# A drain in every expert tile, the row gather ahead of the scale lookup, and the last router block moved

## Chip, core and metric

The kernel runs on one core of a Trainium2 chip. The metric is device time in microseconds (us) for one execution; several executions are taken and their median is given. PE is TensorE, DVE is VectorE, ACT is ScalarE, POOL is GpSimd and SP is SyncE.

## What is computed

Three stages in a row over 2304 tokens of width 512. An attention with features is followed by a gated network, and that by a network of 8 experts of which each token uses one:

```python
def _moe_ref(x, w_gate, w_val, w_out):
    g = x @ w_gate
    silu = g * (1.0 / (1.0 + np.exp(-g)))
    return (silu * (x @ w_val) @ w_out).astype(np.float32)

def _moe2_ref(x, w_gate, w_output_gate, w1, w2):
    logits = x @ w_gate
    e_idx = np.argmax(logits, axis=1)
    ...   # gate_w: the chosen expert's probability; eom: a sigmoid output gate
    for e in range(E):
        mask = e_idx == e
        h = np.maximum(x[mask] @ w1[e], 0.0)
        out[mask] = gate_w[mask, None] * eom[mask, e, None] * (h @ w2[e])
    return out
```

Products are done in single precision by splitting each operand in a high and a low part: three matmuls stand for one product.

## The kernel before

All five engines have a program of their own, written out by hand, and meet through counting semaphores. No scheduler moves anything: an engine executes in the order of the code, and what is behind a waiting instruction waits too.

**The gated network** (`wide`, `narrow`) works on groups of tokens. The last group has 256 tokens, which is two token tiles (t = 0 and 1 of group W = NW). `last_output` (L1588) makes its output, ACT copies it into `y_sb` (`y_copy`, L698), SP stores it into the DRAM tensor `y_rows` (`store_y`, L412), and PE turns it (`turn_y`, L1466) so that the router can use it.

**The router** needs each tile of 128 tokens as three bf16 parts in `y_parts`. ACT makes the first part (`yt_high`, L688). DVE makes the other two in `y_split` (L908): it subtracts the first part (L913, the rest goes back into `y_sb`), casts the rest (L915) and subtracts again (L917). Because L913 overwrites `y_sb`, `y_split` waits on `y_out`, the semaphore of the store. PE then multiplies with the router's weights in `gates` (L1472, matmuls at L1481). After the second tile of the last group DVE chooses experts, counts and places the tokens, and writes a table that says which tokens each expert tile takes.

**The expert tiles.** There are 20 of them here, numbered 0 to 19, of up to 128 tokens each. Tiles 0 and 1 are written out and belong to the largest expert, whose tokens of the earlier groups are known early; tiles from 2 on are loops with the table's numbers. For one tile t, PE does `layer1` in two halves (L1629), turns h (`turn_h`, L1644), turns the rows of the NEXT tile out of the buffer `xg` (`turn_rows(t + 1)`, L1521; in the trace `xg` is a slice of `stage`), and does `layer2` (L1657). The turned rows of tile t + 1 leave `xg` free, and POOL then gathers the rows of tile t + 2.

POOL's loop for tile t (`tile`, L619) is: wait until the scatter of tile t - 1 has landed (`o_out`); look up the scales of tile t, which is two copies (`row_out`, L624, and `scale_row`, L625) and an indirect DMA into `scale_in` (L567); wait for `xt_done` and gather the rows of tile t + 2, which is a copy (`row_in`, L608) and an indirect DMA (L610); wait for `o_ready` and scatter the result of tile t into `out` (L572). There are two such loops. The one for t = 2 to 15 has no drain, the one for t = 16 to 19 has `pool.drain()` (L622) behind its first wait.

DVE's loop for tile t ends with `share(t)`, which on some tiles splits the next expert's weights (`e_lo`, L1154), and `scaled(t)` (L1165): it waits for layer 2 and for the lookup (`sc_in`), then multiplies `bank7` by `scale_in` into `o_sb` (L1172). The next instruction on DVE is `h_low(t + 1, 0)` (L1163), on which layer 2 of the next tile waits on PE.

The weights of the next expert (4 MB, `e_w`) are loaded by SP in eight DMAs when the last tile of the expert before the current one is done.

Of the kernel before, what the change touches and what calls it, by code (L numbers as in the profile page):

```python
# [29 lines left out]
def build(nc, qT, kT, v, v_tail, w_phi, w_gate, w_val, w_out, w_router, w_outgate, w12, out):  # L30
# [28 lines left out]
    WT = WG // P  # L59
    NW = NT // WG  # L60
# [16 lines left out]
    with ExitStack() as ctx:  # L77
        def sb(name, shape, dt=F32, scope=ctx):
            return scope.enter_context(nc.sbuf_tensor(name, shape, dt))

        def sem(name):
            return ctx.enter_context(nc.semaphore(name))
# [76 lines left out]
        silu = sb("silu", [P, 2, GT], F32, m_ctx)  # L159
# [6 lines left out]
        y_sb = sb("y_sb", [P, WT, DM], F32, m_ctx)  # L166
# [72 lines left out]
        y_out = [sem(f"y_out{i}") for i in range(WT)]  # L239
# [42 lines left out]
        o_out = sem("o_out")  # L282
# [26 lines left out]
        def both(x):  # L309

            return x.rearrange("p a n -> p (a n)")
# [22 lines left out]
        def alone(eng, value):  # L334


            value = eng.to_reg(value)
            eng.wait_ge(consts, 6)
            return value
# [148 lines left out]
        def _(pool):  # L488
# [77 lines left out]
            def scale_lookup(rows, n, at):  # L566
                pool.indirect_dma_start(scale_in[:], None, rows, bass.IndirectOffsetOnAxis(ap=at, axis=0),  # L567
                                        bounds_check=n - 1, oob_is_err=False).then_inc(sc_in, 16)

            def scatter(t, rows):  # L570
                pool.wait_ge(o_ready, alone(pool, t + 2))
                pool.indirect_dma_start(out, bass.IndirectOffsetOnAxis(ap=rows, axis=0), o_sb[:], None,  # L572
                                        bounds_check=NT - 1, oob_is_err=False).then_inc(o_out, 16)
# [33 lines left out]
            def gather(t, col):  # L607
                pool.tensor_copy(row_in[:], place_rows[:, bass.ds(col, 1)]).then_inc(ri_ready, 1)  # L608
                pool.wait_ge(ri_ready, alone(pool, t - 1))
                pool.indirect_dma_start(xg, None, y_rows, bass.IndirectOffsetOnAxis(ap=row_in[:, 0:1], axis=0),  # L610
                                        bounds_check=NT - 1, oob_is_err=False).then_inc(xg_in, 16)
# [3 lines left out]
            def gather_ahead(t):  # L615
                pool.wait_ge(xt_done, alone(pool, t + 2))
                gather(t + 2, pool.value_load(table[0:1, bass.ds(t + (T_COL + 2), 1)], min_val=0, max_val=PLACES - 1))

            def tile(t, drained):  # L619
                pool.wait_ge(o_out, alone(pool, t * 16))  # L620
                if drained:
                    pool.drain()  # L622
                col = pool.value_load(table[0:1, bass.ds(t + T_COL, 1)], min_val=0, max_val=PLACES - 1)
                pool.tensor_copy(row_out[:], place_rows[:, bass.ds(col, 1)]).then_inc(ro_ready, 1)  # L624
                pool.tensor_copy(scale_row[:], scale_at[:, bass.ds(col, 1)]).then_inc(sr_ready, 1)  # L625
                pool.wait_ge(ro_ready, alone(pool, t - 1))
                pool.wait_ge(sr_ready, alone(pool, t - 1))
                scale_lookup(scale_rows, NT, scale_row[:, 0:1])
                gather_ahead(t)
                scatter(t, row_out[:, 0:1])  # L630

            gather_ahead(0)
# [198 lines left out]
        def _(dve):  # L831
# [76 lines left out]
            def y_split(W, t, at):  # L908

                dve.wait_ge(y_high, alone(dve, W * WT + (t + 1)))  # L910
                dve.wait_ge(y_out[t], alone(dve, W * 16 + 32))
                y_rest = y_sb[:, t, :]
                dve.tensor_tensor(y_rest, bank[at][:], y_parts[:, 0], ALU.subtract).then_inc(y_rested, 1)  # L913
                dve.wait_ge(y_rested, alone(dve, W * WT + (t + 1)))
                dve.tensor_copy(y_parts[:, 1], y_rest).then_inc(y_parted, 1)  # L915
                dve.wait_ge(y_parted, alone(dve, W * (WT * 2) + (2 * t + 1)))
                dve.tensor_tensor(y_parts[:, 2], y_rest, y_parts[:, 1], ALU.subtract).then_inc(y_parted, 1)  # L917
# [264 lines left out]
            last = (NG - 1) * STEPS_R + STEPS_0 + FIRST  # L1182
# [124 lines left out]
        def _(pe):  # L1307
# [164 lines left out]
            def gates(n, t, at, crossed=False):  # L1472

                if crossed:
                    pe.wait_ge(y_crossed, n * 16 + 48)
                else:
                    pe.wait_ge(y_parted, n * 2 + 2)
                for c in range(KC):
                    for part in range(3):
                        w = (3 - part) * 2 * E  # L1480
                        mm = pe.matmul(bank[at][:, t % TT * 6 * E:t % TT * 6 * E + w], y_parts[:, part, c * P:(c + 1) * P],  # L1481
                                       w_parts[:, c, 0:w], start=(c == 0 and part == 0), stop=(c == KC - 1 and part == 2))
                mm.then_inc(lg_done, 1)

            def route_at(g):
                return (4, 5, 0) if isinstance(g, int) and g in (NG - 3, NG - 1) else (R_BANK, R_BANK, 256)
# [67 lines left out]
            def narrow():  # L1554
                W, g, n = NW, 2 * NW - 2, (NW - 1) * WT
                first_at, second_at = route_at(g)[0], route_at(g + 1)[0]
                for c in range(FC):
                    if c == 1:
                        pe.wait_ge(y_copied, W * WT)
                    if c >= 2:  # L1560
                        pe.wait_ge(silu_done, W * FC + (c - 1))
                    product(bank[last_g[c % 2]], wg_hi, wg_lo, c, GT, () if c else x_waits(W)).then_inc(gate_done, 1)
                    if c >= 2:
                        pe.wait_ge(prod_ready, W * FC + (c - 1))
                    product(bank[last_v[c % 2]], wv_hi, wv_lo, c, GT).then_inc(val_done, 1)
                    if c == 0:
                        turn_y(n, 0, T_BANK)
                    if c == 1:
                        gates(n, 0, first_at)
                        turn_y(n + 1, 1, T_BANK)  # L1570
                    if c == 3:
                        gates(n + 1, 1, first_at)
                        turn_y(n + 2, 2, T_BANK)
                    if c == 4:
                        count_tokens(g)
                    if c == 5:
                        gates(n + 2, 2, second_at)
                        turn_y(n + 3, 3, T_BANK)
                    if c == 6:
                        place(g)  # L1580
                    if c == 7:
                        gates(n + 3, 3, second_at)
                    if c == 8:
                        count_tokens(g + 1)
                    if c == 10:
                        place(g + 1)

                def last_output(t, c0, c1):  # L1588
                    cols = slice(t * P, (t + 1) * P)
                    for c in range(c0, c1):  # L1590
                        if t == 0:
                            pe.wait_ge(lo_ready, W * FC + (c + 1))
                        for i, (h, w) in enumerate(((last_hi(c), wo_hi), (last_hi(c), wo_lo), (last_lo(c), wo_hi))):
                            mm = pe.matmul(bank[4 + t][:], h[:, cols], w[:, c, :],
                                           start=(c == 0 and i == 0), stop=(c == FC - 1 and i == 2))
                    if c1 == FC:
                        mm.then_inc(y_done, 1)

                last_output(0, 0, FC)
                turn_rows(0)  # L1600
                last_output(1, 0, FC // 3)
                turn_y(NW * WT, 0, 6)
                last_output(1, FC // 3, FC)
                gates(NW * WT, 0, 4)

            n_gv = 4 * KC
            n_o = FC * DM // (DFF // 2)
# [17 lines left out]
            def layer1(t, rank, half, k0, k1):  # L1625
                for k in range(k0, k1):
                    at = slice(k * P, (k + 1) * P)
                    for i, (x, w) in enumerate(((xgT_hi, e_hi), (xgT_hi, e_lo), (xgT_lo, e_hi))):
                        mm = pe.matmul(bank[half][:], x[:, at], w_part(w, rank, k * EF + half * 512),  # L1629
                                       start=(k == 0 and i == 0), stop=(k == KC - 1 and i == 2))  # L1630
                if k1 == KC:
                    mm.then_inc(l1_done, 1)
# [31 lines left out]
            pe.wait_ge(elo_ready, HALF)  # L1664
            pe.wait_ge(xt_ready, 1)
            layer1(0, 0, 0, 0, 2)
            pe.wait_ge(placed, NG - 1)
            turn_y(NW * WT + 1, 1, 7)
            layer1(0, 0, 0, 2, KC)
# [83 lines left out]
```

## Time and profile before

| | |
|---|---|
| median of three runs | 869.35 us (865.81 to 873.63) |
| the profiled execution's own time | 866.3 us |
| its span, first to last instruction | 864.3 us |
| granted TensorE clock over the span | 1.000 |
| PE busy | 842.8 us (98%) |
| DVE, ACT, POOL busy | 388.8, 257.2, 208.4 us |
| PE busy in 200 to 500 us | 300.0 of 300 us |
| PE busy in 600 to 612 us | 10.81 of 12 us |
| PE busy in 650 to 800 us | 150.0 of 150 us |
| PE busy in 800 to 850 us | 49.43 of 50 us |

A busy share near 100% means that the engine sets the time of that stretch, and that other engines' work is hidden as long as it keeps the pace. Stretches where PE is not full are where a wait shows in the time. The granted clock is 1.000, which is the 2.4 GHz level, in the whole span.

### The profile page before, as it was taken

What the parts mean: (1) busy time and instruction counts of PE and PEld (TensorE: products, weight loads), DVE (VectorE), ACT (ScalarE), POOL (GpSimd) and SP (SyncE); (2) the same over time, 40 slices, a digit from 0 to 9 for tenths busy, and PEclk for the clock granted to TensorE, in tenths of its full rate; (3) what the DMA queues carried; (4) which work ended last, traced back from release to release, by engine and by line L of the source; (5) the groups of instructions that cost most, each with busy time, mean ns of one, the idle gap of its engine ahead of it and who ended that gap; (6) DMA issues with size and microseconds to landing.
All of it is one profiled execution on the core that took longest, in us unless ns stands there. A gap on an engine that the chain in (4) does not pass through costs nothing.

```text
span 864.3 us, 19003 instructions
## 1 busy us (share of the span) xinstructions
PE 842.8 (98%) x6992; PEld 707.7 (82%) x6993; DVE 388.8 (45%) x770; ACT 257.2 (30%) x387; POOL 208.4 (24%) x334
## 2 busy tenths in 40 slices
PE   8998998999999999999999999999989999999997
PEld 6988897888888888888888888998768888888876
DVE  5777896311133432333323422376774233624522
ACT  4665444111131112212132111325243113413421
POOL 5875300742003110122001010001024222333232
PEclk9999999999999999999999999999999999999999
DMA  9895743511023110412012110106511114215101
GB/s 268 250 256 155 228 154 109 161 30 19 1 98 62 31 31 1 128 30 56 5 73 49 24 24 0 50 2 232 207 49 49 49 36 168 112 43 212 49 30 30
DMA packets 85350, 76.93 MB, mean 89 GB/s; under 512 B 43822, under 2 KB 70062, under 8 KB 85296
## 3 DMA queue, kind: packets, MB, share of 16 engines
q1 hardware_dynamic: 78448, 53.59, 21.2%
q0 software_dynamic: 6560, 22.56, 8.3%
q8 instruction: 39, 0.64, 0.3%
q14 instruction: 15, 0.12, 0.0%
q10 hardware_dynamic: 288, 0.02, 0.0%
HBM read 54.11 MB, written 14.70 MB: 80 GB/s over the span
## 4 chain that ended last, share of the span: by engine, by line
PE 88%; DMA 3%; issue 3%; DVE 3%; POOLq 1%; ACT 1%; SPq 0%; ACTq 0%; POOL 0%; DVEq 0%
PE bank L1440 34%; PE bank L1459 15%; PE bank L1657 10%; PE bank L1629 10%; PE bank L1411 4%; PE bank L1329 4%; PE bank L1356 4%; PE bank L1644 2%; PE bank L1393 1%; DMA e_w<-w 1%; PE bank L1521 1%; DMA stage<-y_rows,row_in 1%; DMA k_sb<-kT 1%; PE bank L1481 1%; DMA y_rows<-y_sb 1%
## 5 line engine op out<-in xcount | busy, mean ns | idle before, releaser
L1075 DVE TENSOR_TENSOR prod<-silu,bank 128x512 f32<-128x512 f32 x48 | 32.9, 686 | 188.5 <-PE bank L1440 188.5
L1440 PE MATMUL bank<-x_hi,wg_hi 128*128 128x512 f32 (+1 forms) x240 | 90.9, 379 | 0.0
L1440 PE MATMUL bank<-x_hi,wg_lo 128*128 128x512 f32 (+1 forms) x240 | 88.4, 368 | 0.0
L1440 PE MATMUL bank<-x_lo,wg_hi 128*128 128x512 f32 (+1 forms) x240 | 88.3, 368 | 0.0
L1440 PE MATMUL bank<-x_hi,wv_hi 128*128 128x512 f32 (+1 forms) x240 | 88.3, 368 | 0.0
L1440 PE MATMUL bank<-x_lo,wv_hi 128*128 128x512 f32 (+1 forms) x240 | 88.3, 368 | 0.0
L1440 PE MATMUL bank<-x_hi,wv_lo 128*128 128x512 f32 (+1 forms) x240 | 88.2, 368 | 0.0
L713 ACT ACTIVATE silu<-bank 128x512 f32<-128x512 f32 x48 | 28.7, 598 | 174.5 <-PE bank L1440 174.5
L1459 PE MATMUL bank<-wo_hi,h_lo 128*128 128x512 f32 x192 | 74.7, 389 | 0.0
L1459 PE MATMUL bank<-wo_hi,h_hi 128*128 128x512 f32 x192 | 74.7, 389 | 0.0
L1459 PE MATMUL bank<-wo_lo,h_hi 128*128 128x512 f32 x192 | 74.7, 389 | 0.0
L707 ACT ACTIVATE h_hi<-prod 128x512 fp32r<-128x512 f32 x48 | 30.3, 632 | 142.0 <-DVE prod L1075 142.0
L1657 PE MATMUL bank<-e_hi,hT_hi 128*128 (+1 forms) x160 | 66.3, 415 | 1.2 <-DVE hT_lo L1163 1.0
L1629 PE MATMUL bank<-e_hi,xgT_hi 128*128 (+1 forms) x160 | 64.4, 403 | 0.2 <-DVE xgT_lo L1158 0.2
L1657 PE MATMUL bank<-e_hi,hT_lo 128*128 (+1 forms) x160 | 62.6, 392 | 0.0
L1629 PE MATMUL bank<-e_hi,xgT_lo 128*128 (+1 forms) x160 | 62.6, 391 | 0.0
L1657 PE MATMUL bank<-e_lo,hT_hi 128*128 (+1 forms) x160 | 62.5, 390 | 0.0
L1629 PE MATMUL bank<-e_lo,xgT_hi 128*128 (+1 forms) x160 | 62.3, 389 | 0.0
L587 POOL COPY x_in<-x_planesT 128x256 uint16<-128x256 uint16 x56 | 24.2, 476 | 157.8 <-DMA x_planesT<-x_planes 157.8
L1163 DVE TENSOR_TENSOR hT_lo<-bank,hT_hi 128x512 fp32r<-128x512 f32 x40 | 27.7, 691 | 63.9 <-ACT hT_hi L790 63.8
L584 POOL COPY x_planes<-x_in 128x256 uint16<-128x256 uint16 x56 | 22.8, 436 | 129.5 <-DMA x_in<-x_rows 127.9
L839 DVE TENSOR_REDUCE amax<-bank 128x8 f32<-128x1024 f32 (+1 forms) x40 | 44.6, 1114 | 20.1 <-PE bank L1329 20.0
(252 smaller groups left out, 1638.1 us busy)
## 6 DMA issues: line engine op xcount, KB each, us to landing
e_w<-w SPq DMA_DIRECT2D x32, 512.0 KB, 5.1
stage<-w_out POOLq DMA_DIRECT2D x16, 384.0 KB, 4.2
y_rows<-y_sb SPq DMA_DIRECT2D x18, 256.0 KB, 2.1
k_sb<-kT SPq DMA_DIRECT2D x16, 256.0 KB, 5.0
v_sb<-v SPq DMA_DIRECT2D x16, 256.0 KB, 4.9
q_sb<-qT SPq DMA_DIRECT2D x16, 256.0 KB, 3.5
x_rows<-x_sb SPq DMA_DIRECT2D x16, 256.0 KB, 3.9
x_in<-x_rows SPq DMA_DIRECT2D x4, 1024.0 KB, 5.6
```

Of the source, the lines that this page charges most:

```text
L707: act.activation(both(h_hi[:, c % 2]), both(prod[:]), ACT.Copy).then_inc(hi_ready, 1)
L713: act.activation(both(silu[:]), bank[G_BANK][:], ACT.Silu).then_inc(silu_done, 1)
L839: dve.tensor_reduce(top, proj, AX.X, ALU.max, apply_absolute_value=True).then_inc(amax_done, 1)
L1075: dve.tensor_tensor(both(prod[:]), both(silu[:]), bank[V_BANK][:], ALU.mult).then_inc(prod_ready, 1)
L1163: dve.tensor_tensor(hT_lo[:, at], bank[6 if half else 3][:], hT_hi[:, at], ALU.subtract).then_inc(ht_ready, 1)
L1329: mm = pe.matmul(acc, src[rows, h, j * P:min((j + 1) * P, S)], phi[rows, :], start=True, stop=True)
L1356: mm = pe.matmul(sums(c, i)[cols, :], feat[:, s, sign, at:at + TAIL], v_sb[:, j, 2 * c + hh, :, a], start=(j == 0 and i in (0, 7)), stop=F ...
L1411: mm = pe.matmul(acc, feat[:, s, sign, half * 512 + i * TAIL:half * 512 + (i + 1) * TAIL], kv_sb[:, b, h // 2 if j < JF else half, sign * ...
L1440: mm = pe.matmul(acc[:, 0:width], w[:, k, cols], x[:, k, 0:width], start=(k == 0 and i == 0), stop=(k == KC - 1 and i == 2))
L1459: mm = pe.matmul(bank[O_BANK + t][:], h[:, c % 2, t // TT, cols], w[:, c, :], start=(c == 0 and i == 0), stop=(c == FC - 1 and i == 2))
L1629: mm = pe.matmul(bank[half][:], x[:, at], w_part(w, rank, k * EF + half * 512), start=(k == 0 and i == 0), stop=(k == KC - 1 and i == 2))
L1657: mm = pe.matmul(bank[7][:], h[:, at], w_part(w, rank, HALF_W + k * DM), start=(k == 0 and i == 0), stop=(k == EC - 1 and i == 2))
```

## The change

Three edits. In POOL's loops every tile now has the drain, and tiles 2 to 15 gather the rows of tile t + 2 first and look up the scales of tile t behind it; tiles 16 to 19 keep the lookup first. In the last group (W = NW), `y_split` writes the rest into the `silu` buffer, which nobody uses any more, and no longer waits for the store; `y_sb` stays as it is. And PE's `gates` for the last group's first tile moves from the end of `narrow` to a place inside expert tile 0, behind the first six matmuls of `layer1`.

```diff
-            def tile(t, drained):
-                pool.wait_ge(o_out, alone(pool, t * 16))
-                if drained:
-                    pool.drain()
+            def look_up(t):
                 col = pool.value_load(table[0:1, bass.ds(t + T_COL, 1)], min_val=0, max_val=PLACES - 1)
                 pool.tensor_copy(row_out[:], place_rows[:, bass.ds(col, 1)]).then_inc(ro_ready, 1)
                 pool.tensor_copy(scale_row[:], scale_at[:, bass.ds(col, 1)]).then_inc(sr_ready, 1)
                 pool.wait_ge(ro_ready, alone(pool, t - 1))
                 pool.wait_ge(sr_ready, alone(pool, t - 1))
                 scale_lookup(scale_rows, NT, scale_row[:, 0:1])
-                gather_ahead(t)
+
+            def tile(t, last):
+                pool.wait_ge(o_out, alone(pool, t * 16))
+                pool.drain()
+                if last:
+                    look_up(t)
+                    gather_ahead(t)
+                else:
+                    gather_ahead(t)
+                    look_up(t)
                 scatter(t, row_out[:, 0:1])
...
                 dve.wait_ge(y_high, alone(dve, W * WT + (t + 1)))
-                dve.wait_ge(y_out[t], alone(dve, W * 16 + 32))
-                y_rest = y_sb[:, t, :]
+                if W < NW:
+                    dve.wait_ge(y_out[t], alone(dve, W * 16 + 32))
+                y_rest = y_sb[:, t, :] if W < NW else both(silu[:])
...
                 last_output(1, FC // 3, FC)
-                gates(NW * WT, 0, 4)
...
             layer1(0, 0, 0, 0, 2)
+            gates(NW * WT, 0, 4)
             pe.wait_ge(placed, NG - 1)
             turn_y(NW * WT + 1, 1, 7)
```

On PE at the end of the last group before, the twelve gate matmuls of its first tile (the first three of them are shown) stood between the last output matmul and the first matmuls of expert tile 0:

```order
L1594 MATMUL bank<-wo_hi,h_y 128x512
L1481 MATMUL bank<-w_parts,y_parts 128x48 [waits y_parted]
L1481 MATMUL bank<-w_parts,y_parts 128x32
L1481 MATMUL bank<-w_parts,y_parts 128x16
...
L1629 MATMUL bank<-e_hi,xgT_hi 128x512 [waits xt_ready,elo_ready]
L1629 MATMUL bank<-e_lo,xgT_hi 128x512
L1629 MATMUL bank<-e_hi,xgT_lo 128x512
...
L1469 MATMUL bank<-ident,y_sb 128x128 [waits y_copied,placed]
```

The same place on PE now (L1601 is the output, L1635 is layer 1, L1488 the gates, L1476 `turn_y`):

```order
L1601 MATMUL bank<-wo_hi,h_y 128x512
L1635 MATMUL bank<-e_hi,xgT_hi 128x512 [waits xt_ready,elo_ready]
L1635 MATMUL bank<-e_lo,xgT_hi 128x512
L1635 MATMUL bank<-e_hi,xgT_lo 128x512
...
L1488 MATMUL bank<-w_parts,y_parts 128x48 [waits y_parted]
L1488 MATMUL bank<-w_parts,y_parts 128x32
L1488 MATMUL bank<-w_parts,y_parts 128x16
...
L1476 MATMUL bank<-ident,y_sb 128x128 [waits y_copied,placed]
```

Six matmuls of layer 1 have moved ahead of the gates; `turn_y` of the second tile stands directly behind the gates.

On POOL, the body of the loop for tiles 2 to 15 before (the drain is not among the listed instructions):

```order
L624 COPY row_out<-place_rows 128x1
L625 COPY scale_row<-scale_at 128x1
...
L567 DMA scale_in<-scale_rows,scale_row 128x1 [waits consts,sr_ready,ro_ready]
...
L617 ISA [waits xt_done,consts]
...
L608 COPY row_in<-place_rows 128x1
...
L610 DMA stage<-y_rows,row_in 128x512 [waits ri_ready,consts]
L572 DMA out<-o_sb,row_out 2304x512 [waits o_ready,consts]
```

The same loop on POOL now (L621 and L622 are the two copies of the lookup):

```order
L617 ISA [waits xt_done,consts]
...
L608 COPY row_in<-place_rows 128x1
...
L610 DMA stage<-y_rows,row_in 128x512 [waits ri_ready,consts]
...
L621 COPY row_out<-place_rows 128x1
...
L622 COPY scale_row<-scale_at 128x1
...
L567 DMA scale_in<-scale_rows,scale_row 128x1 [waits consts,sr_ready,ro_ready]
L572 DMA out<-o_sb,row_out 2304x512 [waits o_ready,consts]
```

The gather and its wait for `xt_done` stand ahead of the lookup, and the scatter directly behind the lookup.

## Rows read from the trace of the kernel before

**Rows 1.** The page, part 1: busy us (share), instructions.
```profile
PE 842.8 (98%) x6992; PEld 707.7 (82%) x6993; DVE 388.8 (45%) x770; ACT 257.2 (30%) x387; POOL 208.4 (24%) x334
```
**Rows 2.** Waits of PE, 500 to 866 us: total us, times, longest.
```profile
PE bank L1521 <- DMA stage<-y_rows,row_in: 1.6, 2, 1.0
```
**Rows 3.** The chain that ended last: start us, us, what.
```profile
598.76 4.78 DMA y_rows<-y_sb
```
**Rows 4.** Timeline of PE: start us, us, operation [idle before <- releaser].
```profile
605.71 0.46 PE L1481 MATMUL bank<-w_parts,y_parts 128*128 128x48 bf16 x12 [0.85 <-DVE y_parts L917]
...
607.49 0.60 PE L1469 MATMUL bank<-ident,y_sb 128*128 128x128 f32 x4
...
611.19 0.46 PE L1481 MATMUL bank<-w_parts,y_parts 128*128 128x48 bf16 x12 [0.34 <-DVE y_parts L917]
```
**Rows 5.** Timeline of DVE at the last group's two splits.
```profile
603.63 0.69 DVE L913 TENSOR_TENSOR y_sb<-bank,y_parts 128x512 f32<-128x512 f32 x1 [1.05 <-DMA y_rows<-y_sb]
...
609.11 0.69 DVE L913 TENSOR_TENSOR y_sb<-bank,y_parts 128x512 f32<-128x512 f32 x1 [1.19 <-ACT y_parts L688]
```
**Rows 6.** Timeline of PE: the turning of rows in tiles 16 and 17.
```profile
815.16 0.60 PE L1521 MATMUL bank<-ident,stage 128*128 128x128 f32 x4
...
828.17 0.65 PE L1521 MATMUL bank<-ident,stage 128*128 128x128 f32 x4 [0.57 <-DMA stage<-y_rows,row_in]
```
**Rows 7.** The chain that ended last, just before that.
```profile
813.80 2.75 DMA out<-o_sb,row_out
...
816.63 4.13 POOLq L622
```
**Rows 8.** Line L622, the drain: ns min/median/max, first and last start.
```profile
L622 POOLq DRAIN  x4: 291/291/4134, 816.6 to 851.7; - x4
```
**Rows 9.** DMA queues between 800 and 866 us: packets, MB, share.
```profile
q0 software_dynamic: 1120, 2.36, 11.4%
```
**Rows 10.** The chain in tiles 10 and 11: PE's pace.
```profile
735.74 4.08 PE bank L1629 x18
...
741.65 0.44 PE bank L1521 x4
...
748.02 4.09 PE bank L1629 x18
```
**Rows 11.** Timeline of POOL: lookups, and one whole drained tile from 826.95.
```profile
648.58 1.68 POOL L567 DMA_INDIRECT scale_in<-scale_rows,scale_row  x1 [0.87 <-POOL scale_row L625]
...
734.76 1.37 POOL L567 DMA_INDIRECT scale_in<-scale_rows,scale_row  x1 [0.87 <-POOL scale_row L625]
...
822.76 1.06 POOL L567 DMA_INDIRECT scale_in<-scale_rows,scale_row  x1 [0.89 <-POOL scale_row L625]
...
826.95 1.01 POOL L572 DMA_INDIRECT out<-o_sb,row_out  x1 [1.03 <-DVE o_sb L1172]
830.87 0.19 POOL L624 COPY row_out<-place_rows 128x1 uint32 x1 [2.92 <-issue]
...
832.06 1.05 POOL L567 DMA_INDIRECT scale_in<-scale_rows,scale_row  x1 [0.88 <-POOL scale_row L625]
833.11 0.20 POOL L608 COPY row_in<-place_rows 128x1 uint32 x1
834.18 1.03 POOL L610 DMA_INDIRECT stage<-y_rows,row_in  x1 [0.87 <-POOL row_in L608]
```
**Rows 12.** Timeline of DVE around the scaled results of tiles 2, 9 and 16.
```profile
648.10 4.63 DVE L1154 TENSOR_TENSOR e_lo<-e_w,e_hi  x4 [1.72 <-ACT e_hi L759]
...
654.99 0.69 DVE L1163 TENSOR_TENSOR hT_lo<-bank,hT_hi 128x512 fp32r<-128x512 f32 x1 [1.60 <-ACT hT_hi L790]
...
738.99 0.75 DVE L1172 TENSOR_SCALAR o_sb<-bank,scale_in 128x512 f32<-128x512 f32 x1 [0.38 <-DMA scale_in<-scale_rows,scale_row]
...
740.93 0.69 DVE L1163 TENSOR_TENSOR hT_lo<-bank,hT_hi 128x512 fp32r<-128x512 f32 x1 [1.19 <-ACT hT_hi L790]
...
825.30 0.75 DVE L1172 TENSOR_SCALAR o_sb<-bank,scale_in 128x512 f32<-128x512 f32 x1 [7.05 <-DMA scale_in<-scale_rows,scale_row]
```

## Prediction

> **What bounds the kernel now.** I read the page's busy shares first: PE is busy for 842.8 us, 98% of the span [rows 1]. No edit takes a matmul away or makes one shorter, so the change can only gain what PE loses to waits, and can only cost what new waits it makes PE suffer. I then read PE's waits in the half of the span that the change touches. The gather of rows holds PE up twice, for 1.6 us together [rows 2]; the timeline of PE shows the router's gates waiting for DVE at 605.71 and 611.19 us, 0.85 and 0.34 us [rows 4]. So the whole prize is about two microseconds in 866, and the question is whether POOL and DVE, which today hide behind PE in the expert tiles, still do so.
>
> **Part 1: the last group's rests in `silu`, its first gates inside tile 0.** The chain of waits shows a store of `y_sb`, 4.78 us long [rows 3], and DVE's L913 idle for 1.05 us until that store has landed [rows 5]. Without the wait L913 can start at 603.63 - 1.05 = 602.58. From L913 to the gates it takes 605.71 - 603.63 = 2.08 us, so the parts are ready at 604.66. PE comes free at 605.71 - 0.85 = 604.86, and now does six matmuls of layer 1 first. From the gates to `turn_y`, gates and six matmuls together take 607.49 - 605.71 = 1.78 us, in either order. So PE finds the parts ready and `turn_y` of the second tile starts at 604.86 + 1.78 = 606.64 instead of 607.49. Either of the two edits would remove most of this wait alone; they do not add up. The gain is 0.85 us by the row, up to 1.0 since the modelled ends of matmuls overlap their successors; I take 0.9.
>
> Does it stay gained? What is late next is the second tile's split. It waits for ACT's part, not for a store [rows 5], and that part follows `turn_y`, so it moves with it. The 0.34 us in front of the second gates [rows 4] stays, because matmuls and split move together. All that follows (choice, places, table, scatter of tile 0, gather for tile 2 and its wait on PE, the larger of the two in [rows 2]) hangs on DVE's chain behind those gates and moves forward by the same 0.9 us. The rest of `y_split` in another buffer costs nothing: same instruction, same shape. Term: -0.9.
>
> **Part 2: the drain.** The drain ran in four tiles: three took 0.29 us and the first 4.13 us [rows 8]. That first one stands in the chain, behind the 2.75 us in which the scatter of tile 15 lands [rows 7], and the gather behind it arrives late: the rows of tile 18 are turned 828.17 - 815.16 = 13.01 us after those of tile 17 [rows 6], where a tile takes 748.02 - 735.74 = 12.28 us [rows 10]. PE loses 0.73 us there. I take the 4.13 us for work that piles up in POOL while no drain is executed (some fifty DMAs since the one ahead of the expert tiles) and 0.29 us for the price where three DMAs lie between two drains. With a drain in each tile the first one of the second loop should cost 0.29, the gather there starts 3.84 us earlier, and the 0.73 us go. Term: -0.73, bounds 0 and -0.73.
>
> **Part 3: lookup behind the gather, tiles 2 to 15.** Nothing is added but the 0.29 us of the drain. What moves: the lookup of tile t starts later by the whole gather, which is from `row_in` to the end of the gather's issue, 834.18 + 1.03 - 833.11 = 2.10 us, with the drain 2.39 us. The gather comes earlier by the lookup, 833.11 - 830.87 = 2.24 us [rows 11]. Behind the lookup stand DVE's scaled result, on DVE's queue h_low of the next tile, and behind that PE's layer 2; on POOL the scatter.
>
> Can POOL keep the pace? One cycle: scatter to first copy with drain 830.87 - 826.95 = 3.92; gather 2.10; first copy of the lookup to its issue 832.06 - 830.87 = 1.19; issue to DVE's scaled result 825.30 - 822.76 = 2.54; scaled result to scatter 826.95 - 825.30 = 1.65 [rows 11, 12]. Sum 11.40 us against PE's 12.28. It fits, with 0.9 us to spare. Before, the landing of the lookup was hidden under the gather's issue.
>
> The first tiles are the tight ones, since POOL enters its loop late. Tile 2: the lookup started at 648.58 [rows 11]; now at 648.58 - 0.9 + 2.39 = 650.07, the scaled result can start at 652.61. It must be done (0.75 us) before h_low of tile 3, 654.99 - 0.9 = 654.09 [rows 12], so it must start by 653.34. 0.7 us are left. The lookup's issue is longer beside DVE's splitting of weights, 1.68 us where the others have 1.06 [rows 11]; with that it still just fits. After that tile POOL gains 0.9 us on PE with each tile.
>
> Tile 9 falls into a load of 4 MB of weights. There the lookup took 738.99 - 734.76 = 4.23 us to the scaled result [rows 11, 12]. It now starts at 736.25, the result at 738.79 with 2.54 us and at 740.48 with 4.23; the limit is 740.93 - 0.9 - 0.75 = 739.28. So 0 to 1.2 us of stall. The load is nearly through by then, which is why I take the price near the lower end. One more load, in tile 14, is like it. Together I take +0.3, bounds 0 and +2.4. The gather of these tiles is ahead of its deadline: PE turns rows 741.65 - 735.74 = 5.91 us into a tile [rows 10].
>
> **Sum.** -0.9 - 0.73 + 0.3 = -1.3 us. The profiled execution took 866.3 us, so the changed kernel under the same conditions takes 865.0. The median of the three runs is 869.35, 3.05 above the profiled one; the forecast for a median is 869.35 - 1.3 = 868.0. The three runs lie 7.8 us apart, so a measurement of this kernel can tell a difference of about 1%, 8.7 us, from no change and hardly less; this one is six times smaller.
>
> **Rivals.**
> *POOL falls behind (slower).* If the lookup behind a 256 KB gather takes as long everywhere as in tile 9, 4.23 us, the cycle is 11.40 + 1.69 = 13.09 us, 0.81 over PE's. Tile 2 is late by 650.07 + 4.23 - 653.34 = 0.96, and the 13 tiles after it lose 0.81 each: 11.5 us, minus 1.6 gained, is 879.2. It decides at 12.28 - (11.40 - 2.54) = 3.42 us from lookup to scaled result. For it: the queue carries the gather first. Against: the gather's issue is over 1.19 us and more before the lookup's, and the one unloaded lookup that I can read took 2.54.
>
> *The long drain belongs to the entry into a loop.* Then 4.13 us come at tile 2 and stay at tile 16, and the edit doesn't do what it says. Tile 2's lookup is later by another 3.84 us: 653.91 + 2.54 - 653.34 = 3.1 us of stall; -0.9 + 3.1 + 0.3 = +2.5, so 871.9. Against it: the drain starts only after the 2.75 us wait [rows 7], which would hide a loading of code, and in 800 to 866 us the only queue with packets is POOL's own, none carries instructions [rows 9]. The Trainium skill ("Runtime: NRT & Kernel Launch", section "Instruction fetch mechanics") says that a taken branch whose target is outside the window held on chip forces a fetch before execution goes on. By that rule this rival's 871.9 would hold; the trace does not agree for this place.
>
> *DVE locks POOL out.* Tiles 2, 9 and 14 have the split of weights on DVE, 4.63 us in one piece at tile 2 [rows 12]. If gather and lookup could not be issued until it ends, at 648.10 + 4.63 - 0.9 = 651.83, then with 1.03 for the gather's issue, 1.19 and 2.54 the result of tile 2 starts at 656.59, 3.3 us late; three tiles give 9.8, minus 1.6: 877.5. Against it: the lookup at 648.58 was issued inside this very piece and was through at 650.26, 0.62 later than usual. [...]
>
> **Chances.** My forecast 0.84; loop entry 0.06; POOL falls behind 0.04; lockout 0.03; something I have not seen, either way, 0.03. Faster by over 1% needs 8.7 us where PE's remaining waits here are about 3 us, so only the scatter of measurements could show it: 0.02. Slower by over 1%: 879.2 and part of 877.5 and the scatter, 0.07. Within 1%: 0.91. The range goes from 864.0 (the forecast less half the scatter of the runs) to 873.5 (loop entry, or both load stalls, with scatter).
>
> **What would show it.** Right: no idle time before L1488's first gates; the two later turnings of rows (tiles 17 and 18) 12.28 us apart; every drain near 0.3 us, that of tile 2 perhaps a little more; in tiles 2 to 15 the scaled result starting less than 3 us after the lookup's issue; PE full from 650 to 850. Wrong: a drain of some microseconds in tile 2, PE waiting for hT_lo in tiles 3, 10 or 15, or tiles longer than 12.28 us throughout.

## The result, and the profile after

The changed kernel is slower. Its median is 871.9 us (867.78 to 878.0, 20 runs), that of the kernel before 868.56 us (864.4 to 873.63, 20 runs); the ratio is 1.0046 with a 95% interval of 1.0028 to 1.0063. By the ratio that is +4.0 us (3.3 by the medians) where -1.3 was forecast.

The profiled execution has a span of 874.6 us against 864.3. Not all of it belongs to the change. The first gather of early rows starts at 593.88 us after and at 587.48 before; these 6.4 us arise ahead of all changed code. From 20 to 200 us this execution has a granted clock of 0.97 on the mean, where the one before has 1.00. So I count from that gather. To the end of the span it is 276.82 us before and 280.72 after: +3.9, close to the +4.0 of the timed runs. All the distances below are counted this way.

The waits of PE in the kernel after (us in total, times, longest):

```profile
PE bank L1663 <- DVE hT_lo L1170: 5.8, 7, 1.4
...
PE bank L1528 <- DMA stage<-y_rows,row_in: 0.9, 1, 0.9
```

The two waits for gathered rows of [rows 2] have become one (0.9 us, tile 1); the one of tile 17 [rows 6] is gone. In their place PE waits for `hT_lo`. Where, the timeline of PE tells (the kernel after; L1488 are the gates, L1663 is layer 2):

```profile
612.25 0.46 PE L1488 MATMUL bank<-w_parts,y_parts 128*128 128x48 bf16 x12
...
616.14 0.46 PE L1488 MATMUL bank<-w_parts,y_parts 128*128 128x48 bf16 x12 [0.18 <-DVE y_parts L924]
...
662.51 0.49 PE L1663 MATMUL bank<-e_hi,hT_hi 128*128 x1 [1.36 <-DVE hT_lo L1170]
...
750.04 0.49 PE L1663 MATMUL bank<-e_hi,hT_hi 128*128 x1 [1.34 <-DVE hT_lo L1170]
...
762.90 0.49 PE L1663 MATMUL bank<-e_hi,hT_hi 128*128 x1 [0.34 <-DVE hT_lo L1170]
...
813.58 0.49 PE L1663 MATMUL bank<-e_hi,hT_hi 128*128 x1 [1.33 <-DVE hT_lo L1170]
...
826.57 0.49 PE L1663 MATMUL bank<-e_hi,hT_hi 128*128 x1 [0.46 <-DVE hT_lo L1170]
```

The first gates have no wait now; before it was 0.85 us [rows 4]. The five waits at layer 2 are in tiles 3, 10, 11, 15 and 16, 4.83 us together. The tiles ahead of them, 2, 9, 10, 14 and 15, are the five of the loops in which DVE splits the next expert's weights (`share`). From tile 3 on PE has no other wait; the other two of the seven for `hT_lo` lie ahead of that (0.45 and 0.51 us) and stand in the kernel before as well (0.47 and 0.50). Layer 2 waits for `h_low`, and that stands on DVE behind `scaled` of the tile before, which waits for the lookup. Here is tile 2 on DVE and on POOL in the kernel after:

```profile
653.08 4.63 DVE L1161 TENSOR_TENSOR e_lo<-e_w,e_hi  x4 [1.71 <-ACT e_hi L765]
661.02 0.75 DVE L1179 TENSOR_SCALAR o_sb<-bank,scale_in 128x512 f32<-128x512 f32 x1 [3.30 <-DMA scale_in<-scale_rows,scale_row]
661.68 0.68 DVE L1170 TENSOR_TENSOR hT_lo<-bank,hT_hi 128x512 fp32r<-128x512 f32 x1
```

```profile
653.31 1.04 POOL L608 COPY row_in<-place_rows 128x1 uint32 x1 [3.51 <-issue]
655.24 1.14 POOL L610 DMA_INDIRECT stage<-y_rows,row_in  x1 [0.89 <-POOL row_in L608]
656.39 0.23 POOL L621 COPY row_out<-place_rows 128x1 uint32 x1
656.57 1.18 POOL L622 COPY scale_row<-scale_at 128x1 uint32 x1
658.65 1.03 POOL L567 DMA_INDIRECT scale_in<-scale_rows,scale_row  x1 [0.89 <-POOL scale_row L622]
...
679.28 1.06 POOL L610 DMA_INDIRECT stage<-y_rows,row_in  x1 [0.89 <-POOL row_in L608]
680.34 0.19 POOL L621 COPY row_out<-place_rows 128x1 uint32 x1
680.47 0.17 POOL L622 COPY scale_row<-scale_at 128x1 uint32 x1
681.52 1.02 POOL L567 DMA_INDIRECT scale_in<-scale_rows,scale_row  x1 [0.88 <-POOL scale_row L622]
```

Two of the three copies, each of one column of 128 words, take 1.04 and 1.18 us while DVE works on `e_lo` (653.08 to 657.71). In a tile without a split, 680 us, the same copies take 0.19 and 0.17.

The ends tell more than the lengths. The split is four operations in a row, so they end at about 654.24, 655.40, 656.55 and 657.71. The copies end at 654.35, 656.62 and 657.75, each 0.04 to 0.11 us behind the operation that was running when it began; the short one of 0.23 us began only 0.16 before such an end. The gather's issue begins at 655.24 and ends at 656.38, which is 0.98 after the end at 655.40.

And the drains of the kernel after (minimum, median, maximum in ns):

```profile
L629 POOLq DRAIN  x18: 291/291/704, 651.6 to 861.9; - x18
```

The 4.13 us of [rows 8] are gone, as forecast; the first drain of the loop takes 0.70.

**The theories.** A: the lookup stands 2.1 us later, and on top of that POOL's copies wait for the DVE operation that is running, so that the scaled result is late in just the tiles with a split. B: the drain in every tile makes POOL late. C: the copies are slow because memory or queue is loaded then, whatever DVE executes.

### The profile page after: what moved, and what is told of

The parts are those of the page before. It is cut to its first block, busy times and chain, and to the rows that moved or that the text cites. A ratio compares the mean times of both kernels' runs of the same rounds, so it can differ in the third digit from the quotient of the medians.

```text
span 874.6 us, 19013 instructions
## 1 busy us (share of the span) xinstructions
PE 848.2 (97%) x6992; PEld 711.8 (81%) x6993; DVE 387.8 (44%) x770; ACT 257.5 (29%) x387; POOL 213.2 (24%) x334
## 4 chain that ended last, share of the span: by engine, by line
PE 80%; DMA 7%; issue 6%; DVE 3%; POOLq 2%; POOL 2%; ACT 0%; SPq 0%; ACTq 0%; DVEq 0%
PE bank L1447 34%; PE bank L1466 15%; PE bank L1663 6%; PE bank L1635 5%; PE bank L1418 5%; PE bank L1336 4%; PE bank L1363 4%; DMA out<-o_sb,row_out 3%; DMA scale_in<-scale_rows,scale_row 2%; PE bank L1601 2%; PE bank L1400 1%; PE bank L1650 1%; DVE o_sb L1179 1%; POOL scale_row L622 1%; DMA k_sb<-kT 1%
## 5 line engine op out<-in xcount | busy, mean ns | idle before, releaser
L1663 PE MATMUL bank<-e_hi,hT_hi 128*128 (+1 forms) x160 | 66.4, 415 | 6.1 <-DVE hT_lo L1170 5.8
L1635 PE MATMUL bank<-e_hi,xgT_hi 128*128 (+1 forms) x160 | 64.4, 402 | 0.2 <-DVE xgT_lo L1165 0.2
L1663 PE MATMUL bank<-e_hi,hT_lo 128*128 (+1 forms) x160 | 62.6, 391 | 0.0
L1635 PE MATMUL bank<-e_hi,xgT_lo 128*128 (+1 forms) x160 | 62.6, 391 | 0.0
L1663 PE MATMUL bank<-e_lo,hT_hi 128*128 (+1 forms) x160 | 62.5, 391 | 0.0
L1635 PE MATMUL bank<-e_lo,xgT_hi 128*128 (+1 forms) x160 | 62.3, 389 | 0.0
L1057 DVE TENSOR_TENSOR h_lo<-prod,h_hi 128x512 fp32r<-128x512 f32 x48 | 36.2, 755 | 36.1 <-ACT h_hi L713 36.1
```

The costliest lines, as they stand in the source:

```text
L1057: dve.tensor_tensor(both(h_lo[:, c % 2]), both(prod[:]), both(h_hi[:, c % 2]), ALU.subtract).then_inc(lo_ready, 1)
L1663: mm = pe.matmul(bank[7][:], h[:, at], w_part(w, rank, HALF_W + k * DM), start=(k == 0 and i == 0), stop=(k == EC - 1 and i == 2))
```

## The experiments

All ratios are to the kernel before. Each variant with a ratio ran 12 times.

**Each part by itself.** The first is the order of gather and lookup without the added drains, from the kernel before:

```diff
             def tile(t, last):
                 pool.wait_ge(o_out, alone(pool, t * 16))
-                pool.drain()
+                if last:
+                    pool.drain()
```

(the diff is against the changed tile loop; the router part is that of before).

> The kernel before with one thing changed: tiles 2 to 15 gather first and look up behind it; no drain is added and the router part is as before. Theory A (the lookup stands 2.1 us later and POOL's small copies stretch to about 1.1 us each beside DVE's splitting of weights, so the scaled result, and with it PE, is late after the five tiles with a split): nearly the whole loss is here, PE waits for hT_lo in five tiles, 4 to 5.5 us together, ratio to the kernel before 1.004 to 1.007. Theory B (the drain in every tile is what makes POOL late): no wait for hT_lo over 0.2 us, ratio within 0.1% of 1.

Measured: 1.0085 (1.0055 to 1.0116), 877.46 us. PE waits for `hT_lo` after the same five tiles: 0.35, 1.31, 0.45, 1.27, 0.48 us, 3.86 together, a little under the expected 4. B falls: these waits need no drain. The ratio is above what I expected. One reason that I had left out: the long drain at tile 16 is still there, now behind a POOL that is already late, and costs 2.44 us instead of 0.57:

```profile
606.50 0.46 PE L1488 MATMUL bank<-w_parts,y_parts 128*128 128x48 bf16 x12 [2.06 <-DVE y_parts L924]
...
837.24 0.66 PE L1528 MATMUL bank<-ident,stage 128*128 128x128 f32 x4 [2.44 <-DMA stage<-y_rows,row_in]
```

(Timeline of PE, this kernel.) The upper line shows something else: with the store's wait in place the first gates waited 2.06 us in this execution, against 0.85 in [rows 4]. The chain that ended last shows why: the store took longer than the 4.78 us of [rows 3].

```profile
598.27 6.06 DMA y_rows<-y_sb
```

From the first early gather to tile 2 this execution took 50.33 us, 2.2 more than the kernel before, and the order of gather and lookup has no part in that. How often it happens in the timed runs (869.81 to 879.62 us) was not measured, so the ratio 1.0085 is not the price of the order alone; the waits are.

**The drain alone.**

```diff
-                if drained:
-                    pool.drain()
+                pool.drain()
```

> The kernel before with one thing changed: the drain in every tile. Theory A: no wait for hT_lo in tiles 3 to 16, the drain of tile 16 falls from 4.13 to 0.29 us and the turning of rows in tile 17 is no longer held up; 0.7 us gained, ratio 0.998 to 1.000. Theory B: PE waits for hT_lo after the tiles with a split, 3 us or more, ratio over 1.003.

Measured: 1.0000 (0.9977 to 1.0022), 869.48 us. The wait of tile 17 went, as A and the forecast have it, and no wait for `hT_lo` came. But a new one came that neither theory named, for the gather, in tile 3. From the timelines of POOL and PE of this kernel:

```profile
648.48 1.23 POOL L623 COPY row_out<-place_rows 128x1 uint32 x1 [3.33 <-issue]
649.66 1.19 POOL L624 COPY scale_row<-scale_at 128x1 uint32 x1
```

```profile
657.50 0.66 PE L1520 MATMUL bank<-ident,stage 128*128 128x128 f32 x4 [1.41 <-DMA stage<-y_rows,row_in]
```

DVE's split starts at 648.44 here. Before, the lookup of tile 2 was issued at 648.58 [rows 11] with its copies already done, 0.6 us ahead of the split [rows 12]. The drain of 0.70 us pushes them into it, where they take 1.23 and 1.19 us, and the gather behind them comes too late. So the drain costs, but by way of the same collision.

**The router part alone, and its two halves.**

```diff
-                dve.wait_ge(y_out[t], alone(dve, W * 16 + 32))
-                y_rest = y_sb[:, t, :]
+                if W < NW:
+                    dve.wait_ge(y_out[t], alone(dve, W * 16 + 32))
+                y_rest = y_sb[:, t, :] if W < NW else both(silu[:])
...
-                gates(NW * WT, 0, 4)
...
             layer1(0, 0, 0, 0, 2)
+            gates(NW * WT, 0, 4)
```

> The kernel before with the silu buffer and the moved gates alone; POOL's loops are as before. Both theories: the distance from the first early gather to the first layer 1 of tile 2 shrinks by 1.4 to 1.6 us as in the changed kernel, nothing else moves, ratio 0.998 to 0.9985.

> The kernel before with the silu buffer and the dropped wait alone. Each router edit does it alone: the first gates have no wait of 0.85 us, tile 2 starts 1.4 to 1.6 us earlier as with both, ratio 0.998. Only both together do it: half of that, 0.7 us or less.

> The kernel before with the moved gates alone, the wait for the store stays. Each alone: as the run with the silu buffer alone, ratio 0.998, as long as the store lands within some 5 us; it fails where the store is later. Only both together: 0.7 us or less.

Measured: both 0.9981 (0.9959 to 1.0004), the buffer alone 0.9978 (0.9956 to 1.0001), the gates alone 0.9988 (0.9965 to 1.0011). In the traces the first layer 1 of tile 2 starts 46.65, 46.80 and 46.84 us after the first early gather, in the changed kernel 46.56. In the kernel before it is 48.12, in the runs with its router part that add drains 47.81 (every tile) and 47.70 (from tile 8 on, below). So either half does it alone, and the part is worth 0.9 to 1.6 us in these traces. In the run with the moved gates alone the store took 4.97 us; whether they suffice beside one of 6.06 us, as in the first run, was not tested. The timed ratios agree, though none of the three intervals excludes 1 by itself.

**The lookup first again**, drains and router part kept:

```diff
-                if last:
-                    look_up(t)
-                    gather_ahead(t)
-                else:
-                    gather_ahead(t)
-                    look_up(t)
+                look_up(t)
+                gather_ahead(t)
```

> The changed kernel with the lookup ahead of the gather in all tiles; drain everywhere and the router part stay. Theory A: all stalls in tiles 3 to 16 are gone, 2.2 us under the kernel before and about 6 us under the changed one, ratio to the kernel before 0.997 to 0.998. Theory B: stalls of some 3 us stay, ratio over 1.

Measured: 0.9997 (0.9973 to 1.0021), 868.49 us. The waits for `hT_lo` are gone, which A expected, and it is some 4 us better than the changed kernel; but two waits for the gather came, 1.40 us in tile 3 and 1.31 us in tile 15, so A's ratio of 0.997 to 0.998 was missed. The copies of tile 14, from POOL's timeline of this kernel (the split starts at 797.10):

```profile
797.31 1.05 POOL L621 COPY row_out<-place_rows 128x1 uint32 x1 [7.76 <-issue]
798.31 1.19 POOL L622 COPY scale_row<-scale_at 128x1 uint32 x1
```

With a drain in every tile, either order pays for the collisions: lookup first delays the gather, gather first delays the lookup.

**Does a copy wait for the operation that DVE executes?** The changed kernel, with each split cut in two:

```diff
-                at = bass.ds(at * CW, CW)
-                dve.tensor_tensor(e_lo[:, at], e_w[:, at], e_hi[:, at], ALU.subtract).then_inc(elo_ready, 1)
+                for piece in range(2):
+                    part = bass.ds(at * CW + piece * (CW // 2), CW // 2)
+                    ins = dve.tensor_tensor(e_lo[:, part], e_w[:, part], e_hi[:, part], ALU.subtract)
+                ins.then_inc(elo_ready, 1)
```

> The changed kernel with each of DVE's splits of weights (128x1024, 1.16 us) cut in two of 128x512; the work is the same. Theory A (a small POOL copy waits until the DVE operation that runs has ended): the copies beside the splits take 0.6 to 0.7 us instead of 1.0 to 1.2, the lookup of tiles 2, 9, 10, 14 and 15 starts about 1 us earlier, and of the 4.8 us that PE waits for hT_lo some 3 us go; ratio to the kernel before 1.001 to 1.003. Theory C (the copies are slow because the memory or the queue is loaded there, whatever DVE executes): the copies stay at 1.0 to 1.2 us and the ratio at 1.004 to 1.005.

Measured: 1.0017 (0.9991 to 1.0044), 869.58 us. DVE and POOL in tile 2 of this kernel, and then PE's waits:

```profile
650.81 4.91 DVE L1162 TENSOR_TENSOR e_lo<-e_w,e_hi  x8 [1.72 <-ACT e_hi L765]
```

```profile
651.02 0.53 POOL L608 COPY row_in<-place_rows 128x1 uint32 x1 [3.51 <-issue]
652.43 1.21 POOL L610 DMA_INDIRECT stage<-y_rows,row_in  x1 [0.89 <-POOL row_in L608]
653.65 0.30 POOL L621 COPY row_out<-place_rows 128x1 uint32 x1
653.90 0.65 POOL L622 COPY scale_row<-scale_at 128x1 uint32 x1
```

```profile
659.36 0.49 PE L1665 MATMUL bank<-e_hi,hT_hi 128*128 x1 [0.50 <-DVE hT_lo L1172]
...
746.24 0.49 PE L1665 MATMUL bank<-e_hi,hT_hi 128*128 x1 [0.67 <-DVE hT_lo L1172]
...
809.25 0.49 PE L1665 MATMUL bank<-e_hi,hT_hi 128*128 x1 [0.98 <-DVE hT_lo L1172]
```

The same bytes are split at the same time (4.91 us of DVE instead of 4.63), and the copy falls from 1.18 to 0.65 us, in step with the length of one DVE operation. An operation now ends every 0.61 us (651.42, then 652.04, 652.65, 653.26, 653.88, 654.49), and the three copies end at 651.55, 653.95 and 654.55, again just behind one. C falls. PE's waits after these tiles fall from 4.83 to 2.15 us.

**One copy more, and one less.** In the lookup of the changed kernel (the declarations of the buffers, and in the second diff a wait that goes with its copy, are left out here):

```diff
+                pool.tensor_copy(spare_row[:], scale_at[:, bass.ds(col, 1)])
```

> The changed kernel with one more small POOL copy ahead of the lookup's DMA, into a buffer that nobody reads. Theory A: in the nine or so tiles without a split it costs 0.13 to 0.2 us of POOL's slack and nothing in the time; in the five tiles with a split it takes 1.1 to 1.2 us if DVE still splits when it comes and the lookup is later by that, up to 4 us more in all, ratio 1.007 to 1.009. Theory C: about the same by its own reasoning in loaded tiles 9 and 14 alone, 1 to 2 us more. If order alone set the loss, and not the copies: under 1 us more.

Measured: 1.0047 (1.0022 to 1.0071), 872.52 us; the five waits add up to 5.48 us, 0.65 more. A's ratio of 1.007 to 1.009 was missed, and 0.65 us lies where I had put the rival that order alone sets the loss (under 1 us), so the sum does not decide between them. The single copies do. The new one took 1.20 us in tiles 10 and 15 (here tile 15) and 0.17 to 0.18 in tiles 2, 9 and 14; in tiles 2 and 9 it began 0.02 us ahead of the end of DVE's last operation.

```profile
817.01 1.20 POOL L624 COPY spare_row<-scale_at 128x1 uint32 x1
```

That fits A's condition (DVE must still be splitting), and goes against C, by which the loaded tiles 9 and 14 should have paid.

```diff
-                pool.tensor_copy(row_out[:], place_rows[:, bass.ds(col, 1)]).then_inc(ro_ready, 1)
-                pool.tensor_copy(scale_row[:], scale_at[:, bass.ds(col, 1)]).then_inc(sr_ready, 1)
+                pool.tensor_copy(both_rows[:], both_at[:, :, bass.ds(col, 1)].rearrange("p a o -> p (a o)")).then_inc(ro_ready, 1)
```

> The changed kernel with the two copies of the lookup made one (two columns of one tensor into two columns of another). Theory A: one wait for DVE is gone where the second copy took 1.15 us; the lookup starts 1.1 us earlier in the tiles with a split, PE's waits for hT_lo fall from 4.8 to about 1 us, ratio 0.999 to 1.001. If the order alone set the loss: 0.13 us per tile, no change that can be told, ratio 1.004 to 1.005.

Measured: 0.9991 (0.9963 to 1.0020), 869.09 us; the waits are 0.35, 1.24 and 1.22 us, in tiles 3, 10 and 15, and none in 11 and 16: 2.81 together. More stayed than the 1 us expected. In tiles 9 and 14 the scatter lands late, under the load of weights (POOL is idle for 8.95 and 8.19 us before `row_in`, in tile 10 for 3.07), and `row_in` still meets the split, with 0.91 and 1.15 us. The changed kernel has the same late scatters, 7.84 and 7.21 us of idle time, so in tiles 10 and 15 PE's waits have two causes that add up: the late scatter leaves POOL no room, and the collisions use more than it has. The fall from 4.83 to 2.81 us with the order unchanged speaks against the rival that order alone sets the loss.

**Both cures at once** (one copy, splits cut in two; otherwise the changed kernel).

> The changed kernel with one copy in the lookup and the splits cut in two. Theory A, ledger by copies: what stands beside a split is 0.4 us for the row copy and 0.3 for the one of the lookup, PE's waits for hT_lo are 0 in tiles 3, 11 and 16 and 0.3 to 0.7 in tiles 10 and 15, 1.2 us or less together; ratio 0.997 to 0.9995. If the order without the collisions costs the most of it: over 2.5 us stay, ratio over 1.001.

Measured: 0.9985 (0.9957 to 1.0014), 867.18 us. One wait for `hT_lo` in tiles 3 to 16 is left, 0.46 us, in tile 15. From tile 2 to the end this execution takes 229.53 us against 228.70 before, although tile 17 gives 0.73 back: 1.6 us are lost where the changed kernel loses 6.2. So the new order, with what is left of the collisions, costs 1.6 us in this execution, and most of the other 4.6 were the long collisions. Part of it is chance: in tile 9 the scatter landed early enough for `row_in` to miss the split (0.18 us).

**How long a drain takes.** The kernel before with the second loop from tile 8 on (one execution, 872.9 us, so it has no ratio), and the kernel before with the router part and a loop of one drained tile, tile 12:

```diff
-            with pool.Fori(2, TILES - 2) as t:
+            with pool.Fori(2, 12) as t:
+                tile(t, False)
+            with pool.Fori(12, 13) as t:
+                tile(t, True)
+            with pool.Fori(13, TILES - 2) as t:
                 tile(t, False)
```

> The kernel before with the second, drained loop from tile 8 on instead of 16. The four lengths seen so far (0.29, 0.70, 3.15, 4.13 us for 3, 8, 38 and 50 DMAs of POOL since the drain before) lie on 0.05 us + 0.082 us per DMA: the drain of tile 8, after 26 DMAs, takes 2.2 us, those after it 0.29. If the length belongs to the entry into a loop: 3 to 4.1 us.

> The kernel before with the router part and one more drain, in tile 12 alone, where DVE splits nothing; no drain in the other tiles to 15, lookup first everywhere. If the drain's length is work that piles up since the drain before: some 2.5 to 3.2 us in tile 12, hidden, and 0.5 to 1.5 us in tile 16, so that the turning of rows in tile 17 is not held up; no new wait of PE; 2.2 us under the kernel before, ratio 0.997 to 0.998. If the length belongs to the entry into a loop: near 4.1 us at tile 12 and at tile 16, and the wait of 0.6 us in tile 17 stays, ratio 0.998 to 0.9985.

The drains of the first and of the second kernel:

```profile
L622 POOLq DRAIN  x12: 291/291/2174, 722.1 to 858.6; - x12
```

```profile
L622 POOLq DRAIN  x5: 291/291/3154, 766.2 to 851.9; - x5
```

2.17 us for 26 DMAs that POOL issued since its drain before, and 3.15 for 38. The loop entry as a cause falls: a loop entered at tile 8 pays 2.17, at tile 12 3.15, at tile 16 4.13, all on the same line. The second kernel took 866.58 us, ratio 0.9972 (0.9947 to 0.9997): in its trace PE has no wait at all from tile 3 to the end. It is faster than both given kernels, and its ratio is the lowest here, though its interval overlaps those of the router part's runs. The first, with a drain in tile 9, met the collision there (1.24 and 1.19 us for the lookup's copies) and had a wait of 1.32 us for the gather in tile 10.

There is one more drain in every kernel here, ahead of the early gathers, behind 32 plain DMAs that POOL issues for the weights. In the kernel before:

```profile
L590 POOLq DRAIN  x1: 2676/2676/2676, 509.1 to 509.1; - x1
```

## Why the prediction was wrong

**The step that failed** is that of part 3, "The lookup's issue is longer beside DVE's splitting of weights, 1.68 us where the others have 1.06; with that it still just fits." It priced the split for the DMA's issue and for nothing else, and it did not ask what the 0.62 us were: the issue had waited for the operation that was running (about 649.26) and ended 1.00 us after it. The two copies that the new order moves beside the split were taken at their length in a quiet tile, inside the 2.10 and 1.19 us that I read from a tile at 830 us, where DVE splits nothing. For tile 2 the forecast put the lookup at 650.07; the trace has 658.65 - 6.40 = 652.25 in the same count. The parts: drain 0.70 instead of 0.29 (+0.41), `row_in` to the end of the gather's issue 656.38 - 653.31 = 3.07 instead of 2.10 (+0.97, of which `row_in` has 0.84), first copy to the lookup's issue 658.65 - 656.39 = 2.26 instead of 1.19 (+1.07); sum +2.45, less some 0.3 by which POOL came to this point ahead of the forecast. I had 0.7 us of room. The scaled result started at 661.02 - 6.40 = 654.62, 1.28 after the limit of 653.34, and PE waited 1.36. ("The others" had not all 1.06 either: [rows 11] has 1.37 for tile 9, also beside a split.) The trace of before had the row that would have told, in tile 10, first POOL, then DVE:

```profile
746.48 1.02 POOL L608 COPY row_in<-place_rows 128x1 uint32 x1
```

```profile
746.23 4.64 DVE L1154 TENSOR_TENSOR e_lo<-e_w,e_hi  x4 [1.65 <-ACT e_hi L759]
```

**The term** of the collision tiles was +0.3 with bounds 0 and 2.4; it measured about +6. I had counted two tiles, by the load of weights; there are five, by the split. Tiles 10 and 15 were taken for quiet. What I feared for tile 9, a lookup slow under the load, did not come: lookup to scaled result took 2.42 us there, not 4.23.

**The rival "DVE locks POOL out"** had the mechanism and not the operations: it held back the DMAs' issues until the end of the whole piece, three tiles, 877.5 us. What is held back is each copy and each issue, by at most the one DVE operation of 1.16 us that is running when it begins. I gave it 0.03 because the issue at 648.58 went through; that row excludes a lockout for the whole piece, not one for an operation. The Trainium skill ("SBUF — State Buffer", section "SBUF: two separate sides") limits the lock, for a DVE operation with two SBUF inputs, to a GpSimd operation that reads SBUF, and says that whichever starts first keeps the ports for the whole instruction. The copies read SBUF, the split has two inputs in SBUF, and the halved operation in place of the whole one gave 0.65 instead of 1.18 us: here the runs agree with it.

**What was right.** The pace: 11.40 us were forecast for POOL's cycle in a quiet tile, and from scatter to scatter (674.14 to 685.49) it is 11.35. The rival that POOL falls behind everywhere therefore stayed away; lookup to scaled result took 2.37 us in tile 2. The long drain was piled-up work, not the loop's entry; its 0.73 us came back. In part 1 the direction and the place were right, and that either edit does it alone; the size was 0.9 to 1.6 instead of 0.9. The waits for `hT_lo` in tiles 3, 10 and 15 were on my own list of signs that the forecast is wrong.

**What was luck.** 871.9 us lies inside the stated range of 864.0 to 873.5, and it is to the decimal what I had written for the rival of the loop entry. Neither says anything for the working: the range reached so high for a drain of 4.13 us in tile 2, and that drain took 0.70.

**The ledger**, counted from the first early gather to the end: up to tile 2 -1.56 (48.12 to 46.56), from there +5.46 (228.70 to 234.16), in sum +3.90. The +5.46 are the 0.73 of tile 17 gained and 6.2 lost; the five waits show 4.83 of them as idle time and 0.17 more stand at `h_sb` in tile 2. The remaining 1.2 are not shown by any wait; that they are the refilling of PE behind each wait was not measured.

## What to carry to other kernels

When an instruction is moved, take its length from a row where it stands beside the same work as in its new place, not from a quiet stretch; a copy of 128 words went from 0.18 to 1.18 us. An engine that keeps the pace on average can still be late in the few tiles that have extra work, and these have to be looked at one by one. If a drain is needed now and then, put it in a tile where nobody waits for that engine.

## What the runs showed of the hardware

A small POOL copy (128x1) that begins while DVE executes an operation with two SBUF inputs (the splits; no other kind was looked at) ends only just behind that operation. Its own length says little: it was 1.0 to 1.24 us where the DVE operation of 1.16 us had just begun, 0.65 at most beside operations of half the size, and 0.23 where the end was near. The 14 traces of this case have 110 such copies beside the splits of the expert loops, and all ended 0.04 to 0.16 us after the end of the operation in which they began (the ends are worked out by dividing a split's time evenly among its operations).

The issue of an indirect DMA is held in the same way, and then takes about its usual length. The 107 issues that began inside a split in these traces ended 0.89 to 1.02 us after the end of the running operation, and an issue beside none takes 1.01 to 1.06. Half of them are therefore only 1.11 to 1.15 us long, because they follow a copy by 0.88 us and so begin some 0.2 us before an end. Those that began near the start of an operation took more: the lookup at 648.58 in [rows 11] 1.68, the longest in any trace 1.99 (run with the gates alone, tile 14). The next operation of the split does not hold an issue that is under way.

Beside an operation whose first input is in PSUM a copy kept its usual length. The copy at 830.87 in [rows 11] took 0.19 us and ended at 831.06, inside this one of DVE (the kernel before):

```profile
830.64 0.69 DVE L1163 TENSOR_TENSOR hT_lo<-bank,hT_hi 128x512 fp32r<-128x512 f32 x1 [0.45 <-ACT hT_hi L790]
```

POOL's drain takes time in proportion to the DMAs that POOL issued since the drain before: 0.291 us after 3, 0.704 after 8, 2.174 after 26, 3.154 after 38, 4.134 after 50. The five lie on 0.05 us + 0.0817 us per DMA; the one after 26 was forecast from the other four, as 2.2 us. The drain of 2.676 us after 32 plain DMAs lies near the line too (2.66). The last of those 32 was issued at 169.3 us and the drain began at 509.1, so 340 us in between did not shorten it, and the time that has passed is not what sets the length. In sum draining often costs a little more than draining once: tiles 2 to 16 of the changed kernel have 0.704 + 14 * 0.291 = 4.78 us, the kernel before has 4.13. What changes is where it lies.
